# Moving the turn of the next x behind the second product in a three-layer attention and MoE kernel, with the first copies, the skipped rounds and the clock filler beside it

## What is computed

```python
q_pool = q.reshape(B, H, S // 2, 2, D).mean(axis=3)          # B=2 H=8 S=1152 D=64
attn = softmax(q_pool @ k.T / sqrt(D)); x = attn @ v          # -> x: 1152 x 512
# layer 0: 8 experts, capacity 288, w1 512x1024, w2 1024x512 for each
e = argmax(x @ w_gate); g = softmax(x @ w_gate)[e]
x = g * (relu(x @ w1[e]) @ w2[e])                             # dropped over capacity
# layer 1: only tokens with x @ w_skip > 0, no capacity
x = x + g * (relu(x @ w1b[e]) @ w2b[e])
```

## Time and profile before

| | |
|---|---|
| median of three runs | 652.73 us (652.5 to 654.78) |
| the profiled execution: its own time | 657.46 us |
| its span, first to last instruction | 655.7 us |
| TensorE busy | 596.4 us (91%) |
| VectorE, ScalarE, GpSimd busy | 318.4, 266.8, 182.1 us |
| mean granted TensorE clock | 0.943 |
| attention / layer 0 / layer 1, about | 0 to 288 / 288 to 475 / 475 to 656 us |

### The profile page before, as it was taken

One profiled execution on the slowest core, in us unless ns is written; L12 is line 12 of the kernel. 1 busy time (PEld: TensorE's weight loads), 2 busy tenths in 40 slices (PEclk: granted clock), 3 DMA queues, 4 the chain that ended last, 5 costly groups with the idle time before them and its releaser, 6 DMA issues.

```text
span 655.7 us, 12149 instructions
## 1 busy us (share of the span) xinstructions
PE 596.4 (91%) x3496; PEld 340.9 (52%) x3497; DVE 318.4 (49%) x666; ACT 266.8 (41%) x439; POOL 182.1 (28%) x166
## 2 busy tenths in 40 slices
PE   7839999999999999959699999999857799999994
PEld 7628777777777777736233333333353233333331
DVE  5425666656665757564336662955574022222222
ACT  4524556565665656510133444442102144433310
POOL 4281734445252640001011111221101022222222
PEclk9878999999999999986799999999957799999998
DMA  4786354453527261005999297662782389961111
GB/s 108 160 297 144 96 105 114 87 131 67 138 60 159 46 229 74 21 18 187 389 395 379 79 343 273 266 264 77 269 270 75 114 307 347 342 197 46 42 48 42
DMA packets 42633, 111.55 MB, mean 170 GB/s; under 512 B 16020, under 2 KB 16020, under 8 KB 41536
## 3 DMA queue, kind: packets, MB, share of 16 engines
q1 hardware_dynamic: 38528, 99.03, 47.7%
q0 software_dynamic: 4080, 12.22, 5.6%
HBM read 102.68 MB, written 12.06 MB: 175 GB/s over the span
## 4 chain that ended last, share of the span: by engine, by line
PE 81%; DMA 6%; DVE 4%; issue 3%; POOL 2%; SPq 1%; ACT 1%; DVEq 1%; POOLq 0%
PE psum L901 39%; PE psum L686 13%; PE psum L700 11%; PE psum L734 8%; PE psum L888 4%; PE psum L762 2%; DMA qraw<-in_q_dram 2%; DMA w1ring<-in_moe_w_dram 1%; DMA w2ring<-in_moe_w_dram 1%; PE psum L746 1%; PE psum L730 1%; PE psum L864 1%; POOL KT L330 1%; ACT probs L986 1%; PE psum L903 1%
## 5 line engine op out<-in xcount | busy, mean ns | idle before, releaser
L901 PE MATMUL psum<-w1ring,XT 128*64 x304 | 141.7, 621 | 13.3 <-issue 6.2
L903 PE MATMUL psum<-wright,XT 128*64 128x512 f32 x304 | 141.7, 621 | 0.0
L901 PE MATMUL psum<-w2ring,HT 128*64 x304 | 134.5, 595 | 3.0 <-DVE wright L315 1.6
L903 PE MATMUL psum<-wright,HT 128*64 128x512 f32 x304 | 134.5, 595 | 0.0
L1148 DVE TENSOR_SCALAR_CACHE_REDUCE probs<-psum 128x1152 f32<-128x1152 f32 x72 | 97.6, 1357 | 74.0 <-PE psum L686 74.0
L686 PE MATMUL psum<-KT,QT 128*128 128x384 f32 x480 | 104.4, 356 | 12.4 <-POOL QT L336 10.3
L986 ACT ACTIVATE probs<-probs,nmax 128x1152 f32<-128x1152 f32 x72 | 90.7, 1260 | 46.4 <-DVE probs L1148 46.4
L686 PEld LDWEIGHTS psum<-KT,QT 128*128 128x128 f32 x480 | 82.5, 193 | 24.3 <-POOL QT L336 10.8
L901 PEld LDWEIGHTS psum<-w1ring,XT 128*64 128x64 f32 x304 | 41.8, 143 | 98.5 <-issue 98.5
L700 PE MATMUL psum<-ident,probs 128*128 128x128 f32 x648 | 83.9, 279 | 3.3 <-ACT probs L986 2.9
L901 PEld LDWEIGHTS psum<-w2ring,HT 128*64 128x64 f32 x304 | 40.1, 137 | 82.2 <-issue 82.2
(11 more groups left out here) (165 smaller groups left out, 623.2 us busy)
## 6 DMA issues: line engine op xcount, KB each, us to landing
w1ring<-in_moe_w_dram SPq DMA_DIRECT2D x64, 512.0 KB
w2ring<-in_moe_w_dram SPq DMA_DIRECT2D x64, 512.0 KB
qraw<-in_q_dram SPq DMA_DIRECT2D x30, 288.0 KB, 7.5
kraw<-in_k_dram SPq DMA_DIRECT2D x14, 576.0 KB, 7.2
V<-in_v_dram SPq DMA_DIRECT2D x8, 576.0 KB, 3.8
moe_in<-zero SPq DMA_DIRECT2D x9, 256.0 KB, 3.0
wnext<-in_next_w_dram SPq DMA_DIRECT2D x1, 2304.0 KB, 16.8
out_dram<-moe_in SPq DMA_DIRECT2D x1, 2304.0 KB, 9.5
```

The costliest lines, as they stand in the source:

```text
L901: pe.matmul(psum[0:GRAIN, b, :], lhs[:, c * P:c * P + GRAIN], left, start=first, stop=last, skip_group_check=True)
L903: return pe.matmul(psum[GRAIN:P, b, :], lhs[:, c * P + GRAIN:(c + 1) * P], wright[k][:, cols], start=first, stop=last, skip_group_check=True)
```

## The change

In the diff's order: `fill_right` can take a wait of its own, which comes after it has read the expert's number. On SyncE the load of w2 of expert 2 for layer 1 moves behind the copy to the output, and that copy now waits also for the tables of layer 1 and its first gathered x. On TensorE identity products are added in the routing (8 before `hot_ready`, 15 after the positions, and 12 in place of 8 after the gates, without the wait for `rows_in_ready`). `turn_x(t + 1)` moves behind `y_product(t - 1)`. Step 1 is written out, and the skipped rounds come last, ahead of the last `y_product`. On ScalarE the fill of w1 comes before `copy_xt`. On VectorE five small operations on the gate values move from before the wait for `pos_ready` to behind the placing; the fill of w2 for tile t + 1 comes before `copy_y(t)`; at each layer's start the w1 fill of tile 1 comes before the w2 fill of tile 0. GpSimd's list isn't touched.

```diff
@@ fill_right
-        def fill_right(eng, copy, k, m, t, filled):
+        def fill_right(eng, copy, k, m, t, filled, free=None):
             slot = eng.snap(ring_slot(k, m, expert))
+            if free is not None:
+                eng.wait_ge(*free)
@@ SyncE
-            load_second(1, 2, 0, 7)
             rest = sp.value_load(tab_n[0][0:1, 0:1], min_val=0, max_val=NSLOT - 2)
+            sp.wait_ge(tables_ready, 2)
+            sp.wait_ge(x_loaded_[1], 16)
             sp.wait_ge(y_stored_[0], rest * 16 + 32)
             sp.dma_start(out, x_dram[1]).then_inc(out_filled, 16)
-            sp.wait_ge(tables_ready, 2)
-            sp.wait_ge(x_loaded_[1], 16)
+            load_second(1, 2, 0, 7)
@@ TensorE
+                keep_busy(8, HID_BANK + 1)
                 pe.wait_ge(hot_ready, m + 1)
...
                 mm.then_inc(pos_ready, 1)
+                keep_busy(15, HID_BANK + 1)
...
                 mm.then_inc(gates_found, 1)
-                pe.wait_ge(rows_in_ready, m + 1)
-                keep_busy(8, HID_BANK + 1)
+                keep_busy(12, HID_BANK + 1)
...
                     hidden_product(t)
-                    turn_x(t + 1)
                     if first:
                         pe.wait_ge(gates_found, m + 1)
                     else:
                         y_product(t - 1)
+                    turn_x(t + 1)
                     turn_hidden(t)
...
-                skipped = (NSLOT - 2) - rest
-                with pe.Fori(1, NSLOT) as i:
-                    with pe.If(i > skipped):
-                        step(nc.s_assert_within(...))
+                step(1)
+                with pe.Fori(2, NSLOT) as t:
+                    with pe.If(t < rest + 2):
+                        step(t)
@@ ScalarE
-                    copy_xt(t + 1)
                     if not isinstance(t, int):
                         fill_right(act, nc.scalar.copy, FIRST, m, t + 1, w1_right_[m])
+                    copy_xt(t + 1)
@@ VectorE: dve.wait_ge(exp_ready, m + 1) and the five operations on
@@ r_sum, gate and r_gcut move from ahead of pos_ready to behind r_place
@@ VectorE
                 def step(t):
+                    fill_right(dve, nc.vector.tensor_copy, SECOND, m, t + 1, w2_right_[m], (y_done_[m], t + (START + 1)))
                     copy_y(m, t)
-                    fill_right(dve, nc.vector.tensor_copy, SECOND, m, t + 1, w2_right_[m])
...
+                fill_right(dve, nc.vector.tensor_copy, FIRST, m, 1, w1_right_[m], (hidden_done_[m], START + 1))
                 fill_right(dve, nc.vector.tensor_copy, SECOND, m, 0, w2_right_[m])
-                dve.wait_ge(hidden_done_[m], START + 1)
-                fill_right(dve, nc.vector.tensor_copy, FIRST, m, 1, w1_right_[m])
```

More of the change, by code:

```diff
@@ L970, in _ @@
                 step(0, first=True)
-                skipped = (NSLOT - 2) - rest
-                with pe.Fori(1, NSLOT) as i:
-                    with pe.If(i > skipped):
-                        step(nc.s_assert_within(pe.snap(1 + ((i + rest + (17 - NSLOT)) & 15)), 1, NSLOT - 1,
-                                                skip_runtime_bounds_check_because="the branch leaves 1 to rest + 1"))
+                step(1)
+                with pe.Fori(2, NSLOT) as t:
+                    with pe.If(t < rest + 2):
+                        step(t)
                 y_product(rest + 1)
@@ L1334, in _ @@
                 hot.then_inc(hot_ready, 1)
[L1336 to L1340, removed]
-                tt(r_gcut[:, 1, 0:n], of(gate), r_gcut[:, 0, 0:n].bitcast(F32), ALU.subtract)
                 if m == 1:
@@ L1377, in _ @@
                                             ).then_inc(placed, 1)
+                dve.wait_ge(exp_ready, m + 1)
+                reduce(of(r_sum), of(r_exp), ALU.add)
+                link(nc.vector.tensor_scalar(of(r_sum), of(r_sum), EPS, None, ALU.add))
+                link(nc.vector.reciprocal(of(gate), of(r_sum)))
+                link(nc.vector.tensor_copy(r_gcut[:, 0, 0:n], of(gate)))
+                tt(r_gcut[:, 1, 0:n], of(gate), r_gcut[:, 0, 0:n].bitcast(F32), ALU.subtract)
                 for i in range(2):
```

## The result

The changed kernel takes 681.56 us (median of four runs, 678.79 to 682.37), beside 653.75 us for the kernel before on the same chip (652.5 to 656.76). The ratio is 1.0404, with a 95% interval of 1.0373 to 1.0435. The prediction was 658.5 us in a range of 646 to 667: slower was the likeliest side, but the kernel lost 27.8 us where 5.8 were forecast. The profiled execution of the changed kernel has a span of 679.8 us, against 655.7. Lines have shifted by two or three: products L904 and L906, turns L891, fills L317, residual gather L608, the add with the residual L1293, `copy_y`'s plain copy L1290.

What follows compares the result with a forecast made beforehand. TensorE, holding 81% of the span, was taken as the bound. Starts -14.0, filler -2.5, layer 0 -1.1, layer 1's rounds +11.5 + 0.6 + 4.0 and end +7.3 made +5.8 on the median 652.73: 658.5 us, range 646 to 667.

Steps and rivals of the forecast that it cites:

- The layer starts: TensorE's gaps before each layer's second w1 product shrink (-4.6 and -5.4 us) and its slow clock goes (2.0 each): -14.0.
- Rival C: Layer 1's start: skipped rounds are not what fills the 6.19 us gap, so 5.4 + 2.0 us stay: 665.9; chance 0.07.
- The filler: Added identity products in the routing hold the clock for each layer's first product: -1.3 us a layer, -2.5 in all.
- The turns side by side: Adjacent turns on TensorE save one change between products and transposes: 0.24 us a round (0.05 to 0.32).
- Layer 0: Eight rounds save 0.24 us each (-1.9) and the last y_product waits longer for copy_y(8) (+0.75): sum -1.1 us.
- Layer 1's rounds: The residual gather, behind the moved turn, stalls w2 products: +11.5 us loaded rounds, +0.6 free rounds, +4.0 clock falls.
- L: Time from the residual gather's issue to its landing: 6.3 us in three loaded rounds, 5.4 in one (3.8 to 6.9).
- F: VectorE's order with the w2 fill ahead of copy_y, making TensorE wait; priced only at layer 0's end, +0.75 us.
- Layer 1's end: y_product(8) waits for tile 7's residual, 8.7 us after the turn (+5.3), at low clock (+2.0): +7.3 us.
- A: Layer 1's residual gathers land early, 3.8 us under weights, and the clock holds: 645.4 us, faster; chance 0.12.
- B: Same wait in layer 1 but smaller: L 5.4 us in all four loaded rounds, no clock falls: 651.8; chance 0.26.
- D: Clock low throughout layer 1's routing, so 5.5 us of the added identity products stick out: 665.3; chance 0.05.

Runs made afterwards that it cites:

- a_residual_first: The changed kernel with the residual gather of tile t - 1 ahead of the x gather in GpSimd's list; 654.91 us, ratio 0.9982.
- d: The changed kernel with turn_x(t + 1) back between the two products; 655.46 us, ratio 0.9995.
- f2_only_starts: The kernel before with only step 1 written out, skipped rounds last, and tile 1's w1 fill ahead of tile 0's w2 fill; 640.74 us, ratio 0.9771.
- h2_more_skips: The kernel before with four more skipped rounds on TensorE ahead of step 1 in each layer; 661.9 us, ratio 1.0111.
- g2_only_filler: The kernel before with only the routing's identity products changed (8, 15 and 12 in place of 8); 653.9 us, ratio 0.9987.
- c_both: The changed kernel with the residual gather ahead of the x gather and copy_y ahead of the w2 fill; 638.26 us, ratio 0.975.
- j_both_no_filler: The changed kernel with residual gather and copy_y put first, and the identity products of the kernel before; 637.37 us, ratio 0.9729.
- e2_only_turn: The kernel before with only turn_x(t + 1) moved behind y_product(t - 1); 706.84 us, ratio 1.0783.
- b_copy_first: The changed kernel with copy_y ahead of the w2 fill again on VectorE, without the early wait; 677.78 us, ratio 1.0356.
- m_clock_hold: The changed kernel with 16 identity products ahead of the w2 product in layer 1's steps 2 to 5; 675.11 us, ratio 1.0311.
- i_both_sp_back: The changed kernel with residual gather and copy_y put first, and SyncE's order of the kernel before; 636.5 us, ratio 0.9712.
- k_both_x_back: The changed kernel with residual gather and copy_y put first, and turn_x(t + 1) back between the products; 642.64 us, ratio 0.9802.

## Why the prediction was right and wrong

**The side and the main mechanism were right**: SyncE's weights, GpSimd's fixed order and the moved turn together delay the residual, and w2 products wait for it. Shown by two ways of undoing it, at GpSimd's list and at TensorE's (a, d: -26.7 and -26.1 us).

**The layer starts: right.** From first to second w1 product the stretches shrank by 7.0 and 7.1 us, and the second product ran at full pace, 6.49 us instead of 8.42 and 8.14, which gives 1.9 and 1.6 more (2.0 each were forecast). Of these 17.6 us 3.6 are the first products at full pace, the filler's term; -14.0 remain, the forecast's term, and f2_only_starts gave -15.2 by itself. Rival C falls with h2_more_skips. One reading was incomplete: in layer 0 the gap was put down to VectorE's fill, and by h2_more_skips the skipped rounds fill it as well; the sum is the same because the change takes both away.

**The filler: -2.5 taken, nothing that timed runs can tell.** Between the two traces it looks right: the first products gained 3.6, and +1.0 and +0.3 stand ahead of them. But three of ten first products run at full pace without the filler, so the step "I take -1.3 a layer" took a gain of one execution for that of all; by its ratio g2_only_filler gains 0.9 us (-2.8 to +1.0), and c_both, which has the filler, is 0.9 us above j_both_no_filler. A gain of 2.5 is at the edge of what the first leaves and against the sign of the second. The five VectorE operations, taken as 0, were timed by no run alone. In the traces the product that finds the rows comes 0.4 and 0.7 us sooner (8.31 and 9.87 us after the stage before it, against 8.70 and 10.56), and the identity products stand between it and the turn.

**The turns side by side: 0.24 forecast, 0.30 measured.** That ScalarE's w1 fill, now ahead of the copy, is hidden was right too; what the prediction didn't say is that the move needs this reorder, without which it costs 1.7 to 1.8 us a round (e2_only_turn).

**Layer 0: the mechanism that was missed.** The forecast was -1.1. The trace has +6.6 from the second w1 product to the turn of the last y, and the clock's 1.9 us counted with the starts lie in that stretch, so +8.5. The step that failed is "at the end `y_product(9)` waits for `copy_y(8)`, which now stands behind four fills": the new order was priced only there, and only by the fill's own 2.70 us. Half of the rest was to be read before, from VectorE in a later round of layer 0, where the fill stood behind `copy_y` (400.04) and its wait cost nothing:

```profile
404.32 0.69 DVE L315 COPY wright<-w2ring 128x1024 f32 x1 [3.60 <-DMA w2ring<-in_moe_w_dram]
```

The fill of the other long round (tile 2) did not wait before: it ran at 354.29 behind an idle time of 0.49. In the changed kernel TensorE was 10 us ahead there by the short start (the w2 product before it at 335.71, against 345.88), and the pieces came from 348.32 to 352.61. An engine that puts such a wait ahead of what TensorE needs passes it on. It did in two rounds, by 3.6 and 4.7 us against their neighbours, 1.7 of it the clock, and the end took another 1.6 for the clock. That copying first removes all of this is shown by b_copy_first and c_both; the same stretch of layer 0 takes 147.3 us in b_copy_first and 158.6 in the changed kernel, so that this order cost 11.3 us where 0.75 had been taken.

**Layer 1's rounds: 16.1 forecast, 25.2 measured**, in three terms of the same sum:
- L was taken as 6.3 three times and 5.4 once (L - 3.2 each: +11.5). Measured: 6.2, 8.0, 8.6 and 5.5, of which the same rule makes +15.5. The upper bound, 6.9, was a landing of before, when the gathers left at another moment beside the weights. The move shifted that moment, so it was no bound: in the four traces with the gather behind the late turn the longest landing is 7.9 to 8.6 us, in the nine others read it is 6.7 to 7.2. In the third round VectorE's fill waited for weights too (567.77 to 573.57), but it was done 1.7 us before the rows landed, so F cost nothing there.
- The clock: two falls at 2.0 were taken, three came, at 1.7, 2.3 and 2.6: 6.6. The 6.4 of m_clock_hold are of that size.
- The path: 5.4 us beside L were taken. GpSimd's issue came 4.05 to 4.43 after the turn and the product 1.37 to 1.53 after the add's start, 0.1 to 0.5 us more in each round; in the three free rounds alone 2.0 us instead of 0.6.

**Layer 1's end: +7.3 forecast, +8.3 measured**, the product 9.28 us after the turn (653.51 to 662.79) where 8.7 was said, and at low clock as said.

**SyncE: 0 forecast, perhaps 1 to 2 us.** The gather of tile 1 lands later, as the bound of +1.5 said: its turn waits 1.94 us (503.42). In c_both it waits 1.49 us; with SyncE's order of before (i_both_sp_back) it follows its product without a pause, and that kernel is 1.8 us below c_both by the medians, but the intervals overlap.

**The rivals.** A and B fell with L, which was 5.5 at the least beside the weights, and with three falls of the clock. C is answered above. D fell too: in the same window of layer 1's routing as the earlier trace rows the granted clock is 0.82, not 0.50, and the added products found room (columns as there):

```profile
475.00:494.00 19.00, 15.66 (x113) 14.87 (x112) 14.12 (x52) 0.75 (x3) 1.05 (x1) 0.82 0.25 85
```

**The sum.** Between the traces the miss is 18.3 us (24.1 - 5.8): 9.6 in layer 0, that is F's 11.3 in place of 0.75, less 0.9 that the turns side by side gave above their forecast; 9.1 in layer 1's rounds; 1.0 at its end; nothing in starts and filler together (-16.5 with the 0.3 that the turns gave in layer 1's first round, against -16.5); less the 1.3 by which attention ended sooner in this execution. The other 3.7 us of the 22 are the kernel before's profiled execution, which lay that much above the median (657.46 against 653.75), while the changed kernel's lay on it (681.62 against 681.56). The forecast had carried a difference of two traces over to the medians; two executions of one kernel differ by as much.

## What to carry to other kernels

Before an operation moves, list every engine whose list waits on it, and what stands behind that wait: here one turn held two gathers in one queue, and changing their order there brought back the loss (a_residual_first); with `copy_y` first as well the change was a gain of 2.5% (c_both). Most of that gain is the short starts, which by themselves gave 2.3% (f2_only_starts); the turns side by side, after which the change is named, are worth 4.4 us, measured with both orders put right (k_both_x_back). Of two operations on one engine, the one that another engine needs goes ahead of the one that can itself wait for a DMA; look for such waits in the whole stretch and not only at its end. A landing time read from the trace is not a bound once its issue moves against a bulk load: here the longest went from 6.9 to 8.6 us.

## What the runs showed of the hardware

- A skipped round of a loop whose body holds this kernel's two products and turns costs TensorE 0.97 us (h2_more_skips), while GpSimd passes five of its own in 1.50 us. Behind the last step they cost nothing that shows (f2_only_starts): the last w2 product of layer 1 still begins 2.79 us after the turns, where its fill is done, though five rounds at 0.97 would be 4.8. Why they are cheaper there no run tells; at the starts TensorE stood waiting for the relu rows just before them, at the end it didn't.
- A gather of 128 rows that lands in 3.4 to 3.5 us in the rounds without weight loads took 5.5 to 8.6 us in the changed kernel's four rounds with 2 MB and more of weights on the way. No run moves the loads alone.
- In the changed kernel's layer 1 a gather's issue on GpSimd mostly takes longer while VectorE is in a fill. All six gathers of x by `idx_x` that began during a fill took 1.21 or 1.22 us, and the one issued with VectorE idle (564.60) 1.05; the two by `rows_in` at its start took 1.01 and 1.12 although a fill was running. An index copy that began during a fill took 0.38 to 0.52 us instead of 0.18 to 0.20.
- TensorE's clock after a pause: behind idle times of 3.33, 5.36 and 5.44 us (530.72, 553.33, 576.65) w2 products took 8.2 to 9.1 us in place of 6.5, their first pairs at the level of 1.2 GHz. Behind idle times near 3 us it went both ways: at 2.4 GHz after 3.37 and 2.78 us (354.59, 597.60), at 1.2 GHz after 2.83 and 2.75 (403.67, 462.71). In m_clock_hold the same two products of layer 0 ran at 2.4 GHz after 2.89 and 2.79, and behind the same wait of 2.1 us the last product is slow in c_both and not in j_both_no_filler. The length of the gap alone doesn't tell. Identity products in the gap kept the granted clock at 1.00 over 65 us (m_clock_hold).
